# Attention steps with the scores first: a new order of TensorE's work in a step, and the mask multiplication ahead of the state update

## What is computed

```python
batch, n_heads, seq, head_dim = (4, 8, 768, 48)
for t in range(S):
    kt, vt, rt = (k[:, :, t], v[:, :, t], r[:, :, t])
    cur = np.einsum('bhd,bhe->bhde', u[None] * kt, vt)
    y[:, :, t] = np.einsum('bhd,bhde->bhe', rt, state + cur)
    state = w[None, :, :, None] * state + np.einsum('bhd,bhe->bhde', kt, vt)
# y becomes x, 3072 tokens of 384 features; the second stage starts with
logits = x @ phi        # phi is 384 x 32
```

## Time and profile before

| | before |
|---|---|
| median of 3 runs | 281.01 us (280.82 to 281.03) |
| profiled execution, its own time | 280.6 us |
| its span, first to last instruction | 278.8 us |
| mean granted TensorE clock | 0.978 |
| TensorE busy (matmuls) | 260.8 us, 94% |
| VectorE busy | 153.2 us, 55% |
| ScalarE busy | 88.7 us, 32% |
| GpSimd busy | 30.5 us, 11% |
| DMA | 55.30 MB, mean 198 GB/s |

### The profile page before, as it was taken

One profiled execution on the slowest core, in us unless ns is written; L12 is line 12 of the kernel. 1 busy time (PEld: TensorE's weight loads), 2 busy tenths in 40 slices (PEclk: granted clock), 3 DMA queues, 4 the chain that ended last, 5 costly groups with the idle time before them and its releaser, 6 DMA issues.

```text
span 278.8 us, 10399 instructions
## 1 busy us (share of the span) xinstructions
PE 260.8 (94%) x4505; PEld 220.9 (79%) x4505; DVE 153.2 (55%) x296; ACT 88.7 (32%) x175; POOL 30.5 (11%) x45
## 2 busy tenths in 40 slices
PE   8989799989999998999999989999999999999992
PEld 8967687877788775433468679999999999999991
DVE  5787488888888876247021487342522524425203
ACT  1224254544555544030220273222222222222200
POOL 3222122222222124000000000000000000000000
PEclk9999799999999999999997799999999999999998
DMA  5975889999999999999804700030030300300303
GB/s 158 331 241 171 256 321 322 394 363 395 385 360 365 319 405 418 423 385 414 364 2 155 298 2 1 0 114 0 0 113 0 113 0 0 113 0 1 114 0 119
DMA packets 16324, 55.30 MB, mean 198 GB/s; under 512 B 1936, under 2 KB 5200, under 8 KB 15408
## 3 DMA queue, kind: packets, MB, share of 16 engines
q1 hardware_dynamic: 13216, 43.90, 42.6%
q10 hardware_dynamic: 3088, 11.14, 10.7%
HBM read 50.32 MB, written 4.72 MB: 197 GB/s over the span
## 4 chain that ended last, share of the span: by engine, by line
PE 81%; DVE 13%; issue 3%; ACT 1%; POOL 0%; DVEq 0%; POOLq 0%
PE ps L1183 12%; PE ps L1182 12%; PE ps L1184 12%; PE ps L920 9%; PE ps L954 6%; DVE pt L669 6%; PE ps L886 5%; DVE pt L666 5%; PE ps L932 4%; PE ps L1167 4%; PE ps L1054 4%; PE ps L1076 4%; PE ps L1023 2%; PE ps L1085 1%; PE ps L1124 1%
## 5 line engine op out<-in xcount | busy, mean ns | idle before, releaser
L1183 PE MATMUL ps<-w2l,hh 128*128 128x384 f32 x192 | 64.5, 336 | 0.0
L1182 PE MATMUL ps<-w2h,hh 128*128 128x384 f32 x192 | 64.4, 335 | 0.0
L821 DVE SCALAR_TENSOR_TENSOR hl<-ps,hh 128x512 fp32r<-128x512 f32 x48 | 32.9, 689 | 57.1 <-ACT hh L567 57.1
L1184 PE MATMUL ps<-w2h,hl 128*128 128x384 f32 x192 | 64.2, 335 | 0.0
L567 ACT ACTIVATE hh<-ps 128x512 fp32r<-128x512 f32 x48 | 28.7, 600 | 74.1 <-PE ps L1167 74.1
L1183 PEld LDWEIGHTS ps<-w2l,hh 128*128 128x128 f32 x192 | 36.0, 188 | 1.6
L1182 PEld LDWEIGHTS ps<-w2h,hh 128*128 128x128 f32 x192 | 36.0, 188 | 0.7
L1184 PEld LDWEIGHTS ps<-w2h,hl 128*128 128x128 f32 x192 | 36.1, 188 | 0.0
L434 POOL TENSOR_TENSOR kt<-intk,kttab 128x384 f32<-128x384 f32 x24 | 24.1, 1006 | 74.7 <-DVE rkb L637 50.0
L637 DVE TENSOR_TENSOR rkb<-ind,tab 128x1024 f32<-128x1024 f32 x24 | 29.9, 1246 | 1.4 <-DMA ind<-dmaj 1.3
L920 PE MATMUL ps<-rkb 64*64 64x128 f32 x768 | 27.5, 279 | 0.0
(11 more groups left out here) (163 smaller groups left out, 308.1 us busy)
## 6 DMA issues: line engine op xcount, KB each, us to landing
ind<-dmaj SPq DMA_DIRECT2D x22, 512.0 KB, 8.0
wearly<-wa ACTq DMA_DIRECT2D x21, 512.0 KB, 7.4
intk<-tmaj SPq DMA_DIRECT2D x24, 384.0 KB, 7.1
wearly<-wa SPq DMA_DIRECT2D x4, 1536.0 KB, 10.0
out<-acc SPq DMA_DIRECT2D x5, 768.0 KB, 3.6
wlate<-wa SPq DMA_DIRECT2D x4, 768.0 KB, 8.3
wlate<-wa SPq DMA_DIRECT2D x2, 1536.0 KB, 10.7
wmid<-wa SPq DMA_DIRECT2D x1, 1536.0 KB, 8.0
```

The source lines that it names most:

```text
L821: v.scalar_tensor_tensor(out=hl[:, f % 4, :], in0=ps[:, f % 4, :], scalar=0.0, in1=hh[:, f % 4, :].bitcast(F32), op0=ALU.max, op1=ALU.subt ...
L1182: mm(o, a_h, w2h[:, f, :], start=(f == 0), stop=False)
L1183: mm(o, a_h, w2l[:, f, :], start=False, stop=False)
L1184: ins = mm(o, a_l, w2h[:, f, :], start=False, stop=(f == KF - 1))
```

## The change

On TensorE, `scores` comes before `increments`; then `turn`; then the logits of batches 0 and 1; then the first carried set; then the logits of batches 2 and 3; then the second carried set; then `within`. The wait for xs moves ahead of `turn`, the wait for stb stays with the first carried set, and so does the wait for the first set with the second. `lg_done` is given by the second half of the logits alone. The number of matmuls is the same. On VectorE the mask multiplication, with its wait for the scores, moves ahead of the update of stb, with its wait for the increments, so that the update stands between the multiplication and the copy.

```diff
@@ VectorE, one step
+                dve.wait_ge(sc_done, n + 1)
+                v.tensor_tensor(pt[:, :, :, :], score[:, :, :, 0, :],
+                                causal, ALU.mult).then_inc(pt_ready, 1)
                 dve.wait_ge(inc_done, n + 1)
                 wait(dve, st_ready, 2 * (n - PAIRS) + 2 + 1 if c else 0)
                 update(stb[0:P, ip, :, :], sta[0:P, ip, :, :], 0)
-                dve.wait_ge(sc_done, n + 1)
-                v.tensor_tensor(pt[:, :, :, :], score[:, :, :, 0, :],
-                                causal, ALU.mult).then_inc(pt_ready, 1)
                 dve.wait_ge(pt_ready, n + 1)
@@ TensorE
-            def logits(ip):
-                for b in range(B):
+            def logits(ip, first=0, end=B):
+                for b in range(first, end):
...
-                ins.then_inc(lg_done, 1)
+                if end == B:
+                    ins.then_inc(lg_done, 1)
...
+                scores(n, ip)
                 increments(n, ip)
-                scores(n, ip)
+                pe.wait_ge(xs_ready, n + 1)
+                turn(n)
+                if ip == 1:
+                    pe.wait_ge(lts_ready, c + 1)
+                logits((ip - 1) % PAIRS, 0, B // 2)
                 pe.wait_ge(st_ready, n * 2 + 1 + 1)
-                pe.wait_ge(xs_ready, n + 1)
                 go()
                 carried(ip, True)
-                turn(n)
+                logits((ip - 1) % PAIRS, B // 2)
                 pe.wait_ge(in_done, n + 1)
                 go()
                 carried(ip, False)
-                if ip == 1:
-                    pe.wait_ge(lts_ready, c + 1)
-                logits((ip - 1) % PAIRS)
                 within(n, ip)
```

## The result

The changed kernel takes 283.17 us, the median of 20 runs (281.28 to 287.20), against 281.03 (277.86 to 284.29, 20 runs) for the kernel before. The ratio is 1.0094, 95% interval 1.0069 to 1.0119. The forecast was 283.3 us in a range of 280.2 to 286.6, with 0.73 on slower. The ratio leaves out runs more than 1.5% above the fastest of their kernel, the medians do not. The profiled execution took 282.45 us, its span is 280.6 (before: 280.6 and 278.8).

The account below looks back on a forecast made before the run. The prediction took TensorE, VectorE, TensorE as the chain before (3.70 us) and VectorE's loop (3.82) as the bound after. Terms +1.9, +0.3, +0.4 and -0.35 gave +2.25 on 280.6, 282.85; 0.4 to the median made 283.3, range 280.2 to 286.6.

Parts of the forecast that it names:

- start to first `within`: Before the steady steps: first scores need not wait for kt, so `within` comes at 14.95 in place of 15.31, -0.35 us.
- plain: Step distances without a branch: 16 of them, each 0.12 us longer, +1.9 us.
- early ones: The first three step distances, with issue gaps and a half-clock stretch: +0.12 us each, +0.4 in all, bounds 0 and 1.0.
- four with a branch: Four later steps where TensorE's loop branches back: each 0.07 us longer, +0.3 in all.
- just covered: First carried set's wait for stb: stb ready 2.32 us after the first score, TensorE there after 2.35, so no delay.
- A: Rival, faster: half-filled logits waves overlap neighbours and shape changes beside 32-column tiles are free; step 3.51, 276.3 us; chance 0.16.
- B: Rival, no change: only the logits halves are cheaper, by 0.11 in the loop's one half; 3.71, 280.9 us; chance 0.12.
- other bound: Lower price for half the logits on TensorE: half the time between the two matmul waves saved, 0.11 us less per half.
- TensorE's own step: TensorE's work from `within` to `within` after the change, shape changes included: 3.77 us.
- VectorE's loop: Mask multiplication, stb update, first set, half logits, second set, sta update, preparation, next mask multiplication: 3.82 us a step.
- The pipe rule (D): Rival on VectorE: the next operation waits until the pipe is empty; loop 4.06, 288.8 us; chance 0.04.
- C: Rival, slower: the second carried set's wait for the first is not hidden behind a half; step 4.01, 287.6 us; chance 0.11.

Follow-up runs that it names:

- e2: The changed kernel with VectorE preparing the rows of step n+2 before the sta update, not after it: step 3.77 us, ratio 1.0025.
- e3: The changed kernel with all logits in one piece between the two carried sets: step 3.93 us, ratio 1.0111.
- e4: The changed kernel with all logits ahead of the first carried set and nothing between the sets: step 3.81 us, ratio 1.0050.

## Why the forecast was right, and where its sum was not

The two pairs of traces, split at the first `within`, at the fifth and at the last (us, changed less before):

| stretch | forecast | first pair | second pair |
|---|---|---|---|
| start to first `within` | -0.35 | -0.14 | -0.39 |
| first four distances | +0.5 | -1.53 | +0.76 |
| other 19 distances | +2.1 | +3.46 | +3.40 |
| last `within` to the end | 0 | +0.08 | -0.19 |
| span | +2.25 | +1.9 | +3.6 |

The forecast's 23 distances are split here as one plain and three early ones, 0.12 + 0.4, and 15 plain and four with a branch, 15 x 0.12 + 0.3.

**Chain before, and what could be won.** Right: once scores go first and VectorE's work overlaps, `within` no longer waits for the copy, which is done at 44.50, 0.48 before `within` (forecast 0.3). Not right: the first set "just covered". That took the mask multiplication to start 1.16 after the first score; with VectorE still on the preparation it starts 1.34 after it (41.51 to 42.85), and the set 0.14 later than the half ahead of it allows.

**Halves.** Right: 0.34 each, measured. The half-filled waves overlap with nothing (rivals A and B out): two matmuls start at 43.52 and two at 43.65, 0.13 apart as in the whole call. The prediction's other bound, 0.11 less for a half, is called half of that distance, which is 0.07. So the 0.11 that both rivals were priced with comes out of no row; their steps would be 3.55 and 3.75 with 0.07, and the halves of 0.34 rule out either.

**Shape changes.** The forecast for TensorE's own step, 3.77, is e2's step to the hundredth, so four changes become five at about 0.1 each holds as a sum. Two places show it by itself: the increments take 0.59 to the start of the transposes (42.40 to 42.99) and 0.47 to the start of the scores, and the second set takes 0.26 to `within` of its own shape (44.72 to 44.98) and 0.37 to the logits (45.02 to 45.39). The Trainium skill (TensorEngine Tiling (Array Packing), Key Properties) says that a change of tiling mode drains TensorE. The traces agree that a change costs time, but they do not show a full drain: in the earlier trace rows the transposes start at 44.49, 0.15 after the start of the last carried matmul and 0.07 before its end as modelled (44.34 + 0.22).

**VectorE's loop.** The mechanism is right and shown by e2 and e3; its size was 3.82 and is 3.91. The term that was mis-sized is "0.22 for that, 0.06 to VectorE": 0.28 from the second set's last matmul to the sta update, measured 0.35 (44.94 to 45.29; 0.34 to 0.35 in e4 too). The 0.06 came from the scores and the mask multiplication; the reaction to the carried set is about 0.13. Where the rest goes is in the chain of e3: VectorE's queue handles the wait of L672 for the carried set as an instruction of its own (53.52 to 53.54), and the update starts 0.04 after that; ahead of the mask multiplication the trace has no such row. That this makes the difference is not shown, as no run took the second wait away. Then 0.33 for 0.31 from update to preparation, and a hundredth or two from set to set. The wait ahead of the sta update is 0.79 for a forecast of 0.6.

**The pipe rule (D).** Out. The stb update starts at 43.45, while the mask multiplication ends at 43.53; the rule as the prediction took it would put it at or after 43.53. But the prediction was wrong to call its rows "against the page": the same section of the Trainium skill (VectorE: DVE Perf Modes, "The DRAIN you can't avoid") goes on: "A next op that is not held starts earlier". These starts 0.08 ahead of the end agree with that sentence. The 0.62 that I took for a pair which the trace of before did not have is 0.60.

**The steady sum.** 2.1 for the last 19 distances, measured 3.4 to 3.5: the 0.09 again, for the 15 plain ones (3.1 for a forecast of 1.8, though the last of them is only 3.77: behind step 22 there is nothing left to prepare); the four with a branch grew by 0.38 for a forecast of 0.3.

**What brought the total back.** In the first pair the kernel before had its half clock in the fifth step and the changed one had none, worth about 1.3 (5.37 against 4.07 in its second trace); the second pair, with no fall among the steps in either, differs by 3.6. That the forecast's 2.25 and the measured 2.14 between the medians (2.6 by the ratio) agree so well is in part luck, as the terms agree less: the loop was 1.3 too small over the last 19 distances, and the first steps and the clock, which differ from run to run by as much, went the other way in part. I cannot say how much of the median's difference each makes. The upper end of the range, 286.6, is called "the half of C"; half of the way from 283.3 to C's 287.6 would be 285.4. The measured time lies inside either.

## What to carry to other kernels

When a wait is taken out of a loop over two engines, follow the instruction that is moved last on the one engine to what is queued behind its waiter on the other: here the late second set held a state update, and behind that 1.2 us of work that had nothing to do with it. A chain that names one engine at 89% does not prove that engine the bound; moving the independent work ahead of the waiter (e2) or taking work off the busy engine (e3) tells. Before you split an operation whose matmuls run side by side in the array's blocks in order to cover a wait, price the half: here it cost nearly the whole, 0.34 of 0.36, more than the 0.17 us that the wait cost bare.

## What the runs showed of the hardware that I had not expected

- A wait of TensorE for its own matmuls, bare, idles it 0.17 us; VectorE's sta update starts 0.35 after the start of the carried set's last matmul, 0.13 after its end, where the mask multiplication starts 0.06 after the end of the scores.
- The 3.4 us stretch at 1.2 GHz comes at different places in executions of the same kernel: at 31 us in one trace, at 108 us in another, with steps of 5.37 and 4.07 us in the place of the first.
